# Loading the first query and key blocks in 512-byte runs and turning them with 64-column identity products

## What is computed

```python
scores = scale * np.matmul(q, k.transpose(0, 1, 3, 2))
mask_plain = (rel >= 0) & (rel < window)                                   # window = 32
mask_dil = (rel >= 0) & (rel < window * dilation) & (rel % dilation == 0)  # dilation = 4
...
attn = attn / (np.sum(attn, axis=-1, keepdims=True) + 1e-09)
return np.matmul(attn, v).astype(np.float32)
...
k = np.maximum(xk @ w_k, 0.0); v = k * k @ w_v; r = 1.0 / (1.0 + np.exp(-(xr @ w_r)))
...
u = x + h.transpose(0, 2, 1); h2 = np.maximum(u @ w_ch1, 0.0) @ w_ch2
```

## Time and profile before

| | us |
|---|---|
| median of 3 runs (698.8 to 700.02) | 699.45 |
| the profiled execution | 700.67 |
| span of the profiled execution, first to last instruction | 698.9 |
| PE busy | 686.7 (98% of the span) |
| DVE busy | 365.9 (52%) |
| ACT busy | 236.3 (34%) |
| POOL busy | 202.4 (29%) |
| DMA, mean rate over the span | 66 GB/s |

### The profile page before, as it was taken

The page is one execution under the profiler, slowest core; times in us unless marked ns, Lnnn a source line. Parts: engine busy times, 40 slices in busy tenths (PEclk is TensorE's granted clock), DMA queues, the critical chain, the costliest instruction groups (busy, mean ns, idle before and its releaser), DMA issues.

```text
span 698.9 us, 14338 instructions
## 1 busy us (share of the span) xinstructions
PE 686.7 (98%) x5777; PEld 612.9 (88%) x5777; DVE 365.9 (52%) x623; ACT 236.3 (34%) x546; POOL 202.4 (29%) x238
## 2 busy tenths in 40 slices
PE   8799999999999999999999999999999999999997
PEld 7678999999999999999888888888788888888886
DVE  5579877686767767786762136231461225411121
ACT  4574553635454453636521122111231122111110
POOL 6374654746464655644063000000000000000000
PEclk9999999999999999999999999999999999999999
DMA  9871233333332331232721311303112221300011
GB/s 198 213 190 38 50 70 55 59 58 56 70 62 48 63 70 32 78 66 66 302 44 26 56 19 61 67 13 65 60 28 42 40 36 61 62 7 1 0 61 31
DMA packets 179729, 45.85 MB, mean 66 GB/s; under 512 B 167880, under 2 KB 172112, under 8 KB 179664
## 3 DMA queue, kind: packets, MB, share of 16 engines
q1 hardware_dynamic: 175424, 43.71, 28.3%
q10 hardware_dynamic: 4240, 1.23, 1.0%
HBM read 30.22 MB, written 4.72 MB: 50 GB/s over the span
## 4 chain that ended last, share of the span: by engine, by line
PE 94%; DVE 2%; ACT 1%; DMA 1%; issue 1%; SPq 0%; POOL 0%; DVEq 0%; ACTq 0%; POOLq 0%
PE bank L956 13%; PE bank L958 12%; PE bank L957 12%; PE tq L956 8%; PE tq L958 8%; PE tq L957 8%; PE s L1528 4%; PE s L1527 4%; PE s L1526 4%; PE bank L1527 3%; PE bank L1528 3%; PE bank L1526 3%; PE bank L1011 2%; PE bank L823 2%; PE s L602 1%; PE s L589 1%
## 5 line engine op out<-in xcount | busy, mean ns | idle before, releaser
L1518 DVE SCALAR_TENSOR_TENSOR h_lo<-bank,h_hi 128x512 fp32r<-128x512 f32 (+1 forms) x30 | 18.9, 637 | 100.7 <-ACT h_hi L1512 100.6
L1518 DVE SCALAR_TENSOR_TENSOR h_lo<-tq,h_hi 128x512 fp32r<-128x512 f32 (+1 forms) x30 | 18.9, 637 | 98.9 <-ACT h_hi L1512 98.9
L1051 POOL TENSOR_TENSOR k_lo<-kr,k_hi 128x288 fp32r<-128x288 f32 x64 | 55.1, 866 | 28.6 <-ACT k_hi L1047 28.4
L1093 DVE RECIPROCAL rg<-rg 128x288 f32<-128x288 f32 x32 | 61.4, 1922 | 0.0
L1512 ACT ACTIVATE h_hi<-tq 128x512 fp32r<-128x512 f32 (+1 forms) x30 | 16.7, 556 | 118.7 <-PE bank L1528 97.0
L1512 ACT ACTIVATE h_hi<-bank 128x512 fp32r<-128x512 f32 (+1 forms) x30 | 16.7, 556 | 118.0 <-PE bank L1528 93.4
L956 PE MATMUL bank<-k_hi,WV_hi 128*128 128x288 f32 x184 | 55.9, 304 | 0.0
L957 PE MATMUL bank<-k_hi,WV_lo 128*128 128x288 f32 x184 | 54.2, 295 | 0.0
L958 PE MATMUL bank<-k_lo,WV_hi 128*128 128x288 f32 x184 | 54.1, 294 | 0.0
L1528 PE MATMUL s<-C_hi,h_lo 128*128 128x512 f32 x120 | 47.6, 396 | 0.0
L1526 PE MATMUL s<-C_hi,h_hi 128*128 128x512 f32 x120 | 47.1, 393 | 0.3 <-DVE urows L1555 0.3
(11 more groups left out here) (242 smaller groups left out, 1987.8 us busy)
## 6 DMA issues: line engine op xcount, KB each, us to landing
C_raw<-in_moe_w_ch SPq DMA_DIRECT2D x6, 1024.0 KB, 11.7
urows<-blocks SPq DMA_DIRECT2D x64, 64.0 KB, 2.1
out_x<-urows SPq DMA_DIRECT2D x16, 256.0 KB, 2.0
vt<-in_v SPq DMA_DIRECT2D x70, 48.0 KB, 2.3
qraw<-in_q SPq DMA_DIRECT2D x128, 24.0 KB, 2.0
kraw<-in_k SPq DMA_DIRECT2D x128, 24.0 KB, 1.9
xraw<-blocks SPq DMA_DIRECT2D x48, 64.0 KB, 2.1
vt<-in_v SPq DMA_DIRECT2D x7, 320.0 KB
```

The costliest lines, as they stand in the source:

```text
L1051: e.tensor_tensor(lo, t, hi.bitcast(F32), ALU.subtract).then_inc(Z.lo_done, 1)
L1093: e.reciprocal(t, t).then_inc(Z.r_done, 1)
L1518: e.scalar_tensor_tensor(lo, ps[:, 0:w], 0.0, hi.bitcast(F32), ALU.max, ALU.subtract).then_inc(Z.h2l_done, 1)
```

## The change

It touches the first four units alone. Both parities of a token pair are now in one descriptor: row m holds, for each of four heads, tokens 2m and 2m + 1, 128 numbers or 512 bytes. A half (four heads) takes one DMA of 96 x 4 descriptors for queries and one for keys, and the tile's second index is the half, no longer the parity. The landing semaphores count 16 in place of 32. Since the parities of one head now lie side by side, and the two heads of a pair 128 columns apart, the turning goes head by head: a plain product of a 64-column block with the identity, whose result goes to PSUM rows 0 to 63 for the pair's first head and to rows 64 to 127 for the second. Units 4 to 7 are loaded and turned as before.

```diff
 def q_landed(n):
-    return ((Z.q_in_a, 32), (Z.q_in_b, 32), (Z.q_in_1a, 32), (Z.q_in_1b, 32))[n] if n < 4 else (Z.q_in, 32 * (n // 2 - 1))
+    return ((Z.q_in_a, 16), (Z.q_in_b, 16), (Z.q_in_1a, 16), (Z.q_in_1b, 16))[n] if n < 4 else (Z.q_in, 32 * (n // 2 - 1))
...
 def load_first(s, half):
-    h0 = 4 * half
+    def load(e, src, dst, landed):
+        b, j, _ = where(2 * s)
+        e.dma_start(dst.rearrange("p (h x) -> p h x", h=4),
+                    src[b, 4 * half:4 * half + 4, SU * j:SU * (j + 1), :].rearrange("h (m u) d -> m h (u d)", u=2))\
+            .then_inc(landed, 16)
     def sync(e):
-        for u in range(2):
-            load_rows(e, q, s, raw_q(s, u), u, h0, 4, (Z.q_in_a, Z.q_in_b, Z.q_in_1a, Z.q_in_1b)[2 * s + half])
+        load(e, q, raw_q(s, half), (Z.q_in_a, Z.q_in_b, Z.q_in_1a, Z.q_in_1b)[2 * s + half])
...
 (transposes, for s and u in range(2))
+    if n < 4:
+        for h in range(2):
+            c0 = P * (2 * s + h) + D * u
+            last = e.matmul(dst[D * h:D * (h + 1)], raw(n // 2, dil)[:, c0:c0 + D],
+                            ident[0:2 * QB, 0:2 * QB], start=True, stop=True)
+        continue
     c0 = P * (2 * dil + s)
     last = e.transpose(dst, raw(n // 2, u)[:, c0:c0 + P],
                        ident[0:2 * QB, 0:2 * QB])
```

More of the change, by code:

```diff
@@ L358, in q_landed @@
         def q_landed(n):
-            return ((Z.q_in_a, 32), (Z.q_in_b, 32), (Z.q_in_1a, 32), (Z.q_in_1b, 32))[n] if n < 4 else (Z.q_in, 32 * (n // 2 - 1))
+            return ((Z.q_in_a, 16), (Z.q_in_b, 16), (Z.q_in_1a, 16), (Z.q_in_1b, 16))[n] if n < 4 else (Z.q_in, 32 * (n // 2 - 1))
         def k_landed(n):
-            return ((Z.k_in_a, 32), (Z.k_in_b, 32), (Z.k_in_1a, 32), (Z.k_in_1b, 32))[n] if n < 4 else (Z.k_in, 32 * (n // 2 - 1))
+            return ((Z.k_in_a, 16), (Z.k_in_b, 16), (Z.k_in_1a, 16), (Z.k_in_1b, 16))[n] if n < 4 else (Z.k_in, 32 * (n // 2 - 1))
         def raw_v(n, rows, h, heads=1):
@@ L386, in load_first @@
         def load_first(s, half):
-            h0 = 4 * half
+            def load(e, src, dst, landed):
[3 more added lines that the diff above has]
+                    .then_inc(landed, 16)
             def sync(e):
-                for u in range(2):
-                    load_rows(e, q, s, raw_q(s, u), u, h0, 4, (Z.q_in_a, Z.q_in_b, Z.q_in_1a, Z.q_in_1b)[2 * s + half])
+                load(e, q, raw_q(s, half), (Z.q_in_a, Z.q_in_b, Z.q_in_1a, Z.q_in_1b)[2 * s + half])
             def scalar(e):
-                for u in range(2):
-                    load_rows(e, k, s, raw_k(s, u), u, h0, 4, (Z.k_in_a, Z.k_in_b, Z.k_in_1a, Z.k_in_1b)[2 * s + half])
+                load(e, k, raw_k(s, half), (Z.k_in_a, Z.k_in_b, Z.k_in_1a, Z.k_in_1b)[2 * s + half])
             return dict(sync=sync, scalar=scalar)
```

## The result

The changed kernel takes a median of **704.75 us** over 4 runs (702.55 to 705.63), the kernel before 699.49 us over 4 runs on the same chip (698.8 to 700.02). The ratio is 1.0067, 95% interval 1.005 to 1.0084: **slower by 5.3 us**, and outside the range of 698.0 to 702.6. The profiled execution takes 704.54 us with a span of 702.7; before it was 700.67 and 698.9. So of the 5.3 us between the medians the profiles show 3.9.

A forecast was written before the change was run, and what follows sets the result against it. The prediction took TensorE, busy for 98% of the span, as the bound, with all to win or lose in the first 31 us. A 2.3 us delay less 2.2 recovered gave +0.1 on 699.45, rounded to 699.5 us, range 698.0 to 702.6.

The forecast's parts named there:

- PE starts turning when its keep-warm products are through; no turning waits for data: Start of the prologue: data land before PE turns them, so the faster loads at once shorten nothing.
- the step of +0.66: Turning of units 0 to 3: 32 instructions at 0.041 us, 1.32 us a unit against 0.66, four times +2.64.
- The clock was granted in full throughout: Reading of the profile before the change: PE's clock was full over the whole span; no us were set for it.
- the rival of halves one after another: Turning products do not run side by side: 703.8 us in full, 700.4 in part; chance 0.17.
- The hole: PE's 0.99 us stop in `scores(3)`, read as a late instruction block; it moves to `scores(2)`, leaving PE 2.0 late, not 2.64.
- The next block: The following instruction block falls into `weighted_values(0)` near 19 us and costs 0.3 us of waiting, up to 1.3.
- +0.1: Whole sum on the profiled execution: 2.3 us lost in the prologue less 2.2 us come back.
- S: Delay of the first feed-forward products: 2.3 us later, within 1.3 to 3.3.
- What comes back: Waits for WK's last quarter and the keys of n = 4: 2.2 of 2.36 us regained through earlier loads.
- the key load is no quicker: Rival at the keys of n = 4: SP stays stuck by its own descriptors, +2.3, 701.8 us; chance 0.13.
- the median is 1.2 below that execution, and on it the forecast is 699.45 + 0.1: Last step: the sum from the profiled execution of 700.67 us is put on the median, rounded to 699.5 us.

The follow-up runs named there:

- square at full clock: Medians at full clock, idle stretch filled: old loads 698.61 us with old transposes, 700.96 with 64-column products; new loads 698.20 and 701.86.
- e3: The changed kernel with eight keep-warm products in place of seven before the first turning: median 704.67 us, 701.34 in its executions at full clock.
- e5: The changed kernel with six keep-warm products in PE's idle stretch before the values of unit 1: median 701.86 us.
- e7: The changed kernel with eight keep-warm products at the start and six before the values of unit 1: median 702.09 us.
- e2: The kernel before with the new 64-column products but its old 256-byte loads: median 705.29 us.
- e1: The changed kernel with the new loads but the old 128-column transposes, so values differ from the reference: median 700.99 us.
- e9: e1 with four keep-warm products before the values of unit 1: median 700.37 us, 698.20 in its executions at full clock.
- e6: The kernel before with four keep-warm products before the values of unit 1: median 698.67 us, 698.61 in its executions at full clock.
- e10: e2 with six keep-warm products before the values of unit 1: median 701.13 us, 700.96 in its executions at full clock.
- e4: The kernel before with plain 128-column products in place of the transposes in units 0 to 3: median 705.88 us.
- e12: e6 without the 11 keep-warm products between turning and scores: median 701.91 us.

## Why the prediction failed, step by step

Two steps failed. The sum had no term for the clock, which goes with 2.9 us; and it credited the median with 2.2 us of waits won back, which were read in one execution slower than the median. In the square at full clock the new loads give 0.4 us with the old turning and take 0.9 with the new one, while the products cost 2.35 to 3.7.

**"PE starts turning when its keep-warm products are through; no turning waits for data": right in form, wrong in speed.** Unit 0 starts at 5.17, but its 32 instructions take 2.71 us where the later units take 1.47, and e3, one keep-warm product longer, turns it in 1.47. Before, unit 0 took 0.80 us (5.04 to 5.84). So the step of +0.66 was +1.85 here. Products at about half the pace are what the lower level of the clock would give, but the granted clock of the stretch is 1.00, so that is argued from the pace. "The clock was granted in full throughout" is what the column says of the kernel before, and I took it as a property that the change would inherit. The pace of unit 0 is the outcome of one execution: the change and e5 are one program up to there, and leave unit 0 at 7.88 and 7.49 us; e3 and e7 are too, and take 1.47 and 2.24 us for it (5.60 to 7.84 in e7).

**+0.66 us a unit by two halves side by side: right in kind, 0.1 too small.** From turning to keep-warm, units 1 to 3 take 1.47 us (9.28 to 10.75, 12.33 to 13.80, 16.59 to 18.06). In the long group of unit 1's queries 16 instructions take 0.71, 0.044 each, near the forecast 0.041 and far from the serial 0.083; in the trace they start in pairs, 0.01 us apart, a pair every 0.08 us. So the rival of halves one after another falls. The Trainium skill, page TensorE: Matmul & The Clock Gate, Part 3: Packing small matmuls, lets a weight load overlap running matmuls only where the row groups differ; all these products are on the same 96 rows, and the serial time that the prediction drew from that rule didn't come. What I left out is the joint where half-width products follow full-width ones and the reverse, about 0.15 us a unit: 1.47 less 32 x 0.041 = 1.31. The units cost 0.77, 0.78 and 0.78.

**The hole: placed rightly, sized wrongly.** I said it would stand 12 matmul instructions into `scores(2)`; it stands behind 14, at the 220th matmul of the trace against the 218th before. But I had the block arrive near 14.2 and the hole shrink by 0.64 us. PE went on at 16.13, after 1.12 us of idling. One packet of instructions passes between 13 and 15 us, and none from 11 to 13, where it was before. The queue of TensorE's instructions from 13 to 15 us:

```profile
q8 instruction: 1, 0.02, 4.3%
```

The runs show whose doing that is. With the old loads and the new products (e2) the packet passes between 11 and 13 us and the hole is gone, more than I forecast. With the new loads and the old turning (e1, e9) it is 2.16 and 2.77 us long at an unchanged count of 218. Slices of 0.2 us of the DMA view place the packet:

| | loads, turning | packet from (us) | PE stops | goes on |
|---|---|---|---|---|
| before | old, old | 11.8 | 14.11 | 15.10 |
| e6 | old, old | 11.4 | 14.12 | 14.99 |
| e1 | new, old | 13.6 | 14.32 | 16.48 |
| e9 | new, old | 14.2 | 14.19 | 16.97 |
| e2 | old, new | 11.0 | no stop | |
| e10 | old, new | 10.8 | no stop | |
| the change | new, new | 13.2 | 15.01 | 16.13 |
| e5 | new, new | 12.4 | 14.63 | 15.20 |
| e7 | new, new | 13.0 | 14.96 | 15.89 |
| e3 | new, new | 12.2 | 13.91 | 14.77 |

PE goes on 2.6 to 3.6 us behind the packet each time, and doesn't stop where the packet came more than 3 us ahead of the 220th matmul (near 14.2 to 14.3 in e2 and e10). e4 and e12, which reach the count elsewhere, fit too: in e12 the packet comes from 16.0 us, 3.6 ahead of the 218th matmul, and nothing stops there; in e4 it comes from 14.0, about 2.3 ahead, and the turning of n = 3, in which the count falls, takes 2.18 us for the 1.86 of the others. In the four pairs that differ by the loads alone (e1 and before, e9 and e6, the change and e2, e5 and e10) the packet comes 1.6 to 2.8 us later with the new ones. So the faster loads themselves hold the instructions up. Why was not tried; that they share the DMA engines, which I argued from, would let me expect the reverse, since the queues drain sooner. The rule cited from the Trainium skill's page Runtime: NRT & Kernel Launch, Instruction fetch mechanics, that such a crossing is mostly hidden, would have the hole be something else, in a fixed place. It kept to the count of 218 or 220 matmuls while its place in the program moved (`scores(3)` before, `scores(2)` in the change, e3, e5 and e7), and was 0.57 to 2.77 us long in eight traces, so the trace disagrees here.

**The next block, 0.3 us: didn't happen.** PE works from 18.93 through `weighted_values(0)` without such a hole. In its place came one that I hadn't seen: **the softmax of n = 1 lost its cover**. It ran beside the hole in `scores(3)`; now it stands before the mask of n = 3 and delays it by 0.56 us, which makes PE's idle stretch 0.37 us longer.

**The clock: the step that failed most.** No term and no rival had it. Behind the idle stretch of 1.52 us the clock falls for 3.4 us in the profiled execution (1.57 us of time) and in e2 for some 10. Filling that stretch brought 2.9 us of median back (e5). With the slow pace of unit 0 (1.2 us over the forecast, and the clock only by its pace) that is most of what the profile shows beyond +0.1. S, forecast at 2.3 within 1.3 to 3.3, came to 6.12.

**What comes back: 2.2 forecast, 2.28 measured, by other shares.** The stop at WK's last quarter cost more than its 1.45 us of idle time: the query turning of n = 4 stands 5.51 us behind the first feed-forward product before (24.20 to 29.71), 3.56 now, so 1.95 came back. Idle time in the trace counts from a modelled end. Of the wait for keys only 0.33 came back: their start is 1.14 us behind that of the queries, 1.47 before. I expected them 5.6 us behind their issue. They were there 6.95 behind it (28.07 to 35.02), and 7.9 behind the first query issue, beyond the 7.3 from which the rival "the key load is no quicker" was to decide; its price of 2.3 us, though, was not paid: from its first issue the load took 7.9 us where it had taken 9.55 (21.63 to 31.18), and WK gave 1.95. In e3 both terms are there nearly whole: S = 3.27 (27.47 less 24.20) and 3.02 back, leaving 0.25 us. So in that execution the balance of the prologue is close to the +0.1 that I gave, but by luck: the loss was 0.97 us more than forecast and the recovery 0.8 more, and the two errors cancel.

**And yet e3 at full clock takes 701.34 us, not 699.5.** That is the second wrong step: "the median is 1.2 below that execution, and on it the forecast is 699.45 + 0.1". The waits that the change can win back were read in an execution that was slower than the median by 1.2 us. e6 shows the same: its profiled execution waits 1.98 us for WK and keys and takes 700.24, the faster ones take 698.5. If the waits are mostly absent from the faster executions of the old form, there is less to recover there than in the profile, and the missing 1.5 to 2 us would be explained. An estimate speaks for it: an execution of 698.5 us has a span of 696.7, and with 668.0 us behind the keys of n = 4, as in e6's trace, PE turns them at 28.7; without any wait that would be 28.0 (24.09 and the 3.94 us of e9), so 0.7 us of waiting fits in, not 1.98. But the prologue ahead of 24.09 may have been quicker as well. Kernels without these waits don't settle it: e5 and e10 show no such distance (701.45 in the profile and 701.86 in the median, 700.84 and 700.96), while e9 does (699.55 against 698.20 at full clock), and so does e7 (703.11 against 702.09). A profiled execution can be slow for other reasons, then, and what the others wait for is argued, not shown: only one execution of each kernel has a trace. (The stated range, too, ends at 702.6, a little short of the 702.8 that the slow key load has at its upper end.) What is shown is the square: at full clock the products cost 2.35 us with the old loads.

**Open:** why the new loads delay the instruction packet; what sets the pace of unit 0, where the granted clock is 1.00 and the spacing is not that of full speed; what the executions without a trace wait for; and e4's time at full clock. No version with the reference's values beat the kernel before: e6, its fill, is equal to it within the interval, and the new loads with the 128-column transposes turn other values (e1, e9).

## What to carry to other kernels

A prologue whose fillers keep the clock up runs on a margin, and an idle stretch longer by 0.37 us went with 2.9 us of clock here: look at every idle stretch that an edit lengthens, and at every chain of another engine that the old stall had covered, and try a filler before judging the edit. Credit for waits recovered is taken from one profiled execution; where that one is slower than the median, the credit is probably too large. A stall without a semaphore that sits at a fixed instruction count keeps to that count when the program around it changes, and its length changed with the loads ahead of it, so an edit of the loads must be costed there too.

## What the runs showed of the hardware that was not expected

- **Half-width float32 products on the same 96 rows** ran at 0.044 to 0.046 us apiece for 96 columns, in groups that write alternating halves of the result, two starting at a time; full-width ones took 0.116 (e4), more than twice that, and the transpose form 0.083.
- **A filler in one idle stretch decides most executions' clock.** At 0.999 or over: of the change none of 4 without and 11 of 11 with 1.6 us of it (e5). It is not a rule: the same filler gave 8 of 11 on the old loads (e10), and one of 1.2 us gave 10 of 11 in e6 and 4 of 11 in e9, which has a hole of 2.77 us elsewhere.
- **512-byte pieces move faster.** From 3 to 5 us, with the change:

```profile
DMA packets 1186, 0.58 MB, mean 290 GB/s; under 512 B 52, under 2 KB 1186, under 8 KB 1186
```

against 219 GB/s for 256-byte ones. That was as expected. That PE's instructions come 1.6 to 2.8 us later behind them, in four pairs of kernels, was not.
